# Expert passes of a mixture-of-experts kernel: the first product of small tiles turned round, and the weights of both layers split as two streams

## The chip, the cores and the metric

The kernel runs on one core of a Trainium2 chip. The metric is the device time of the kernel in microseconds; what is compared is the median of several runs.

## What is computed

Three stages, one after another. Attention over windows of 32 queries gives x of 3072 tokens by 512 features. A mixture of experts follows: tokens with x @ w_skip > 0 go through one of 8 experts, the others are left as they are. The last stage takes the largest of three products and multiplies again. The change is in the second stage:

```python
def _moe_ref(x, w_skip, w_gate, w1, w2):
    do_compute = x @ w_skip > 0
    xc = x[do_compute]
    e_idx = np.argmax(xc @ w_gate, axis=1)          # w_gate: 512 x 8
    ...
    for e in range(E):                               # E = 8
        mask = e_idx == e
        h = np.maximum(xc[mask] @ w1[e], 0.0)        # w1[e]: 512 x 1024
        y[mask] = gate_w[mask, None] * (h @ w2[e])   # w2[e]: 1024 x 512
    out[do_compute] = xc + y
```

## The kernel before

Tokens are sorted by expert into tiles of at most 256 tokens (`TOK`). A tile of at most 128 tokens (`P`) is *small*; small tiles come first. With these inputs there are eight tiles: two small ones (passes 0 and 1) and six of 256 (passes 2 to 7). A pass is `tile_pass(i, tokens)`, which every engine has for itself, in a loop over small tiles, in a loop over the large ones, and once more written out for the last tile, where the transposes and sums of the final stage are interleaved.

The precision of fp32 is kept with three products of a rounded part and a rest: `three` issues lo\*hi, hi\*lo and hi\*hi. So every operand is split: ScalarE (ACT) copies it to the reduced type fp32r (`w_hi<-raw`, line 837; `h_hi<-ps_h`, line 851; `x_hi<-ps_x`, line 841), and VectorE (DVE) subtracts that from the original (`w_lo<-raw,w_hi`, line 1215; `h_lo`, line 1267; `x_lo`, line 1222).

A pass has eight feature blocks of 128 hidden features. The weights of block c are one chunk of 128 x 1024 numbers, 512 KB: 512 columns of w1 and 512 of w2. SyncE (SP) loads chunks into a ring of four buffers `raw`; a load waits until DVE has split the chunk four before it. ACT writes the high part when the chunk has landed and TensorE (PE) has used the block four before (`s_used`). The first product of block f (`first_product`) holds w1 in PE and streams the tokens of x past: 4 x 3 matmuls with 128 or 256 columns, result `ps_h`, features by tokens. The second (`second_product`) holds a block of h and streams 512 columns of w2 past: three matmuls for each 128 tokens, result `ps_y`. PE runs one block ahead: first product of f+1, then second product of f. Near the end of a pass PE transposes the x rows of the next tile (`turn`, eight transposes, result `ps_x`).

At the end of a pass DVE adds the result to the old rows (`sums_out`, `x_out<-ps_y,g_nat,x_nat`, line 1279). GpSimd (POOL) waits for that sum (`s_xo`), copies the rows of the next tile (`x_nat<-x_in`, line 656, 128 x 1024 within SBUF), and then issues the gathers of the tile after it and the scatter of the sums.

Of the kernel before, what the change touches and what calls it, by code (L numbers as in the profile page):

```python
# [14 lines left out]
P = 128  # L15
# [38 lines left out]
CHK = KD * P + DM  # L54
RAW = 4
RING = 4
LEAD = 3
# [46 lines left out]
def build(nc, qT, kT, vW, w9, wpack, wunit, wout, out):  # L104
# [8 lines left out]
    with ctx:  # L113
# [54 lines left out]
        with ExitStack() as moe:  # L168
            sb, ps = tensors(moe)

            w_hi = [sb(f"w_hi{i}", [P, CHK], F32R) for i in range(RING)]
            w_lo = [sb(f"w_lo{i}", [P, CHK], F32R) for i in range(RING)]
            raw = sb("raw", [P, RAW, CHK])
# [7 lines left out]
            sb("last_stage", [P, (7 * 2 * KH * HT + UBUF * 8 * KH * P + 2 * 7 * KH * P)])  # L181
# [102 lines left out]


# [68 lines left out]

        s_load = [sem(f"s_load{i}") for i in range(RAW)]
        s_whi = sem("s_whi")
        s_wlo = sem("s_wlo")
# [54 lines left out]
        def w1_part(w, k):  # L412
            return w[:, k * P:(k + 1) * P]

        def w2_part(w):
            return w[:, KD * P:]
# [22 lines left out]
        def _(sp):  # L439
# [42 lines left out]
            def load_chunk(e, c, split=None):  # L482
                if split is not None:
                    sp.wait_ge(s_wlo, split)
                sp.dma_start(raw[:, c % RAW, :], wpack[bass.ds(e, 1), c].rearrange("a p c -> (a p) c"))\
                    .then_inc(s_load[c % RAW], 16)

            for c in range(LEAD):
                load_chunk(e0, c)
# [3 lines left out]
            sp.dma_start(gate_dram.rearrange("(p t) o -> p (t o)", p=P), gate[:, :]).then_inc(s_gst, 16)  # L493
            def load_pass(i):
                e_now = sp.value_load(table[0:1, bass.ds(i, 1)], min_val=0, max_val=E - 1)
                e_next = sp.value_load(table[0:1, bass.ds(i + 1, 1)], min_val=0, max_val=E - 1)
                for c in range(LEAD, FB):
                    load_chunk(e_now, c, i * FB + c + 1)
                for c in range(LEAD):
                    load_chunk(e_next, c, i * FB + FB + c + 1)  # L500
# [9 lines left out]
            for c in range(LEAD, FB):  # L510
                load_chunk(e_last, c, last * FB + c + 1)

            for n in range(2, UBUF):
                load_unit(n)
# [275 lines left out]
        def _(act):  # L790
# [42 lines left out]
            def split_w(i, c):  # L833

                act.wait_ge(s_load[c % RAW], i * (16 * FB // RAW) + 16 * (c // RAW + 1))
                act.wait_ge(s_used, i * FB + c + 1)
                act.activation(w_hi[c % RING][:, :], raw[:, c % RAW, :], ACT.Copy).then_inc(s_whi, 1)  # L837

# [5 lines left out]
            for c in range(LEAD):  # L844
                split_w(0, c)
            act.wait_ge(s_tr, 1)
            split_x(P)

            def hidden_high(i, f, tokens):
                act.wait_ge(s_h, i * FB + f + 1)  # L850
                act.activation(h_hi[f % 2][:, 0:tokens], ps_h[f % 2][:, 0:tokens], ACT.Relu).then_inc(s_hhi, 1)

            def tile_pass(i, tokens):
                for f in range(FB):
                    hidden_high(i, f, tokens)
                    if f == FB - 1:
                        act.wait_ge(s_tr, i + 2)
                        split_x()
                    if f + LEAD < FB:
                        split_w(i, f + LEAD)  # L860
                    else:
                        split_w(i + 1, f + LEAD - FB)

            with act.Fori(0, small) as i:
                tile_pass(i, P)
            unit_high(0)
            with act.Fori(small, rest + SPARE - 1) as i:
                tile_pass(i, TOK)
# [124 lines left out]
            for f in range(FB):  # L993
                hidden_high(last, f, TOK)
                if f + LEAD < FB:
                    split_w(last, f + LEAD)
# [39 lines left out]
        def _(dve):  # L1036
# [155 lines left out]
            dve.sem_inc(s_wlo, RAW)  # L1192
# [20 lines left out]
            def split_w(i, c):  # L1213
                dve.wait_ge(s_whi, i * FB + c + 1)
                dve.tensor_tensor(w_lo[c % RING][:, :], raw[:, c % RAW, :], w_hi[c % RING][:, :].bitcast(F32),  # L1215
                                  ALU.subtract).then_inc(s_wlo, 1)
# [28 lines left out]
            split_w(0, 0)  # L1245
            split_w(0, 1)
            unit_sums(0)
            split_x(0, P)

# [15 lines left out]
            def hidden_low(i, f, tokens):  # L1265
                dve.wait_ge(s_hhi, i * FB + f + 1)
                dve.scalar_tensor_tensor(out=h_lo[f % 2][:, 0:tokens], in0=ps_h[f % 2][:, 0:tokens], scalar=0.0,
                                         in1=h_hi[f % 2][:, 0:tokens].bitcast(F32), op0=ALU.max, op1=ALU.subtract)\
                    .then_inc(s_hlo, 1)

            def sums_out(i, tokens):
                dve.wait_ge(s_nat, i * 2 + 2)
                dve.wait_ge(s_landed, i + 1)
                for t in range(tokens // P):
                    if t == 0 and tokens > P:
                        dve.wait_ge(s_y, i + 1)
                    else:
                        dve.wait_ge(s_used, i * FB + FB + RING)
# [4 lines left out]
            def tile_pass(i, tokens):  # L1283
                for f in range(FB):
                    hidden_low(i, f, tokens)
                    if f == FB - 1:
                        split_x(i + 1)
                    elif f + LEAD < FB:
                        if f == 0:
                            split_w(i, LEAD - 1)  # L1290
                        split_w(i, f + LEAD)
                    else:
                        split_w(i + 1, f + LEAD - FB)
                sums_out(i, tokens)

            with dve.Fori(0, small) as i:
                tile_pass(i, P)
            with dve.Fori(small, rest + SPARE - 1) as i:
                tile_pass(i, TOK)
# [135 lines left out]
            for f in range(FB):  # L1435
                hidden_low(last, f, TOK)
                if f == 0:
                    split_w(last, LEAD - 1)
                if f + LEAD < FB:
                    split_w(last, f + LEAD)  # L1440
# [36 lines left out]
        def _(pe):  # L1477
# [146 lines left out]
            def first_product(i, f, tokens):  # L1624
                pe.wait_ge(s_wlo, i * FB + f + 1 + RAW)
                pe.wait_ge(s_hlo, i * FB + f + 1)
                for k in range(KD):
                    if f == 0 and k % (KD // 2) == 0:
                        pe.wait_ge(s_xlo, i * 2 + k // (KD // 2) + 1)
                    last = three(ps_h[f % 2][:, 0:tokens], w1_part(w_hi[f % RING], k), w1_part(w_lo[f % RING], k),  # L1630
                                 x_hi[:, k, 0:tokens], x_lo[:, k, 0:tokens], k == 0, k == KD - 1)
                last.then_inc(s_h, 1)

            def second_product(i, f, tokens):
                pe.wait_ge(s_hlo, i * FB + f + 3)
# [12 lines left out]
            def tile_pass(i, tokens):  # L1648
                first_product(i, 0, tokens)
# [187 lines left out]
```

## Time and profile before

| what | us |
|---|---|
| median of 3 runs | 673.04 (672.7 to 674.03) |
| the profiled execution | 675.65 |
| its span, first to last instruction | 673.9 |
| attention and routing, up to the first expert matmul | 121.57 |
| expert passes 0 to 7 | 121.57 to 304.50 |
| final stage | 304.50 to 673.90 |

The profiled execution took 675.65 us, 1.75 us more than its span. The granted TensorE clock is 1.000 over the whole span. Line numbers are those of the kernel before. A matmul in the trace has a modelled duration that is longer than the distance to the next one; how fast PE goes is read from the distance between starts.

### The profile page before, as it was taken

What the parts mean: (1) busy time and instruction counts of PE and PEld (TensorE: products, weight loads), DVE (VectorE), ACT (ScalarE), POOL (GpSimd) and SP (SyncE); (2) the same over time, 40 slices, a digit from 0 to 9 for tenths busy, and PEclk for the clock granted to TensorE, in tenths of its full rate; (3) what the DMA queues carried; (4) which work ended last, traced back from release to release, by engine and by line L of the source; (5) the groups of instructions that cost most, each with busy time, mean ns of one, the idle gap of its engine ahead of it and who ended that gap; (6) DMA issues with size and microseconds to landing.
All of it is one profiled execution on the core that took longest, in us unless ns stands there. A gap on an engine that the chain in (4) does not pass through costs nothing.

```text
span 673.9 us, 13069 instructions
## 1 busy us (share of the span) xinstructions
PE 651.8 (97%) x4864; PEld 542.4 (80%) x4864; DVE 460.1 (68%) x820; ACT 318.9 (47%) x504; POOL 174.6 (26%) x210
## 2 busy tenths in 40 slices
PE   4999989999999999999999999999999999999998
PEld 3778865788997999988888888888888888888886
DVE  4778867877666656798899873378889516888500
ACT  4445442556544555564455453345456424445311
POOL 7411222476675375405300012100000220000000
DMA  8999964767675587713601115121101111110011
GB/s 301 410 328 341 344 232 175 262 233 265 199 245 166 180 298 248 234 41 119 214 32 63 62 48 188 47 64 62 63 32 63 59 67 52 44 63 32 0 63 62
DMA packets 32505, 101.07 MB, mean 150 GB/s; under 512 B 6012, under 2 KB 6156, under 8 KB 32336
## 3 DMA queue, kind: packets, MB, share of 16 engines
q1 hardware_dynamic: 26288, 87.12, 37.6%
q0 software_dynamic: 6176, 13.41, 5.7%
q8 instruction: 25, 0.41, 0.2%
q14 instruction: 16, 0.13, 0.1%
HBM read 87.11 MB, written 16.80 MB: 154 GB/s over the span
## 4 chain that ended last, share of the span: by engine, by line
PE 89%; DVE 4%; DMA 2%; issue 2%; ACT 1%; another core or an unknown queue 1%; SPq 1%; DVEq 0%; ACTq 0%
PE ps_c L1620 9%; PE ps_c L1622 9%; PE ps_c L1621 8%; PE ps_b L1622 5%; PE ps_b L1620 5%; PE ps_b L1621 5%; PE ps_s L1490 4%; PE ps_h L1620 4%; PE ps_h L1622 4%; PE ps_h L1621 4%; PE ps_o L1505 4%; PE ps_y L1620 3%; PE ps_y L1621 3%; PE ps_y L1622 3%; PE ps_f L1622 2%; PE ps_f L1620 2%
## 5 line engine op out<-in xcount | busy, mean ns | idle before, releaser
L1215 DVE TENSOR_TENSOR w_lo<-raw,w_hi 128x1024 fp32r<-128x1024 f32 x64 | 79.5, 1254 | 42.1 <-ACT w_hi L837 33.7
L837 ACT ACTIVATE w_hi<-raw 128x1024 fp32r<-128x1024 f32 x64 | 67.8, 1060 | 47.6 <-PE ps_y L1622 26.2
L1238 DVE TENSOR_TENSOR u_lo<-u_f,u_hi 128x1792 fp32r<-128x1792 f32 x27 | 54.6, 2023 | 50.3 <-ACT u_hi L826 50.3
L1620 PE MATMUL ps_c<-c_hi,u_lo 128*128 128x512 f32 x216 | 85.2, 394 | 0.6
L1622 PE MATMUL ps_c<-c_hi,u_hi 128*128 128x512 f32 x216 | 84.2, 390 | 0.0
L1621 PE MATMUL ps_c<-c_lo,u_hi 128*128 128x512 f32 x216 | 84.2, 390 | 0.0
L1620 PE MATMUL ps_h<-x_hi,w_lo 128*128 128x256 f32 (+1 forms) x256 | 71.5, 279 | 1.7 <-DVE w_lo L1215 0.9
L1622 PE MATMUL ps_h<-x_hi,w_hi 128*128 128x256 f32 (+1 forms) x256 | 71.9, 281 | 0.0
L1621 PE MATMUL ps_h<-x_lo,w_hi 128*128 128x256 f32 (+1 forms) x256 | 71.9, 281 | 0.0
L777 POOL DMA_INDIRECT out<-f_out,order x16 | 17.6, 1100 | 207.5 <-ACT f_out L792 206.9
L792 ACT ACTIVATE f_u<-ps_c 128x512 f32<-128x512 f32 x58 | 34.6, 597 | 69.8 <-PE ps_c L1622 67.5
L826 ACT ACTIVATE u_hi<-u_f 128x1792 fp32r<-128x1792 f32 x27 | 46.0, 1702 | 27.8 <-PE ps_c L1622 26.0
L1620 PEld LDWEIGHTS ps_h<-x_hi,w_lo 128*128 128x128 f32 x256 | 48.9, 191 | 6.3 <-DVE x_lo L1222 2.5
L1620 PEld LDWEIGHTS ps_c<-c_hi,u_lo 128*128 128x128 f32 x216 | 40.5, 188 | 13.2 <-ACT f_p L792 4.2
L1621 PEld LDWEIGHTS ps_h<-x_lo,w_hi 128*128 128x128 f32 x256 | 48.9, 191 | 2.0
L1622 PEld LDWEIGHTS ps_h<-x_hi,w_hi 128*128 128x128 f32 x256 | 48.9, 191 | 0.0
L1620 PE MATMUL ps_y<-w_hi,h_lo 128*128 128x512 f32 x112 | 46.1, 412 | 1.7 <-issue 1.3
L1622 PEld LDWEIGHTS ps_c<-c_hi,u_hi 128*128 128x128 f32 x216 | 40.6, 188 | 8.6
L1621 PEld LDWEIGHTS ps_c<-c_lo,u_hi 128*128 128x128 f32 x216 | 40.6, 188 | 8.1
L1621 PE MATMUL ps_y<-w_lo,h_hi 128*128 128x512 f32 x112 | 44.1, 394 | 0.0
L1622 PE MATMUL ps_y<-w_hi,h_hi 128*128 128x512 f32 x112 | 43.8, 391 | 0.0
L1621 PE MATMUL ps_b<-c_lo,u_hi 128*128 128x512 f32 x108 | 42.0, 389 | 0.0
(240 smaller groups left out, 1504.3 us busy)
## 6 DMA issues: line engine op xcount, KB each, us to landing
raw<-wpack SPq DMA_DIRECT2D x64, 512.0 KB
u_f<-wunit SPq DMA_DIRECT2D x27, 512.0 KB, 3.3
v_sb<-vW SPq DMA_DIRECT2D x32, 390.0 KB, 5.3
k_sb<-kT SPq DMA_DIRECT2D x32, 250.0 KB, 4.9
q_sb<-qT SPq DMA_DIRECT2D x16, 384.0 KB, 6.0
x_dram<-x_buf SPq DMA_DIRECT2D x4, 1536.0 KB, 10.2
f_in<-x_dram SPq DMA_DIRECT2D x1, 2048.0 KB, 9.0
out<-f_out SPq DMA_DIRECT2D x8, 256.0 KB, 2.0
```

The costliest lines, as they stand in the source:

```text
L777: pool.indirect_dma_start(out=out[0:LISTED, :], out_offset=bass.IndirectOffsetOnAxis(ap=order[:, n:n + 1], axis=0), in_=f_out[:, t % OUTS, ...
L792: return act.activation(dst, src, ACT.Copy)
L826: act.activation(u_hi[n % 2][:, :, :], u_f[n % UBUF][:, 1:8, :], ACT.Copy).then_inc(s_uhi, 1)
L837: act.activation(w_hi[c % RING][:, :], raw[:, c % RAW, :], ACT.Copy).then_inc(s_whi, 1)
L1215: dve.tensor_tensor(w_lo[c % RING][:, :], raw[:, c % RAW, :], w_hi[c % RING][:, :].bitcast(F32), ALU.subtract).then_inc(s_wlo, 1)
L1238: dve.tensor_tensor(u_lo[n % UBUF][:, 1:8, :], u_f[n % UBUF][:, 1:8, :], u_hi[n % 2][:, :, :].bitcast(F32), ALU.subtract).then_inc(s_ulo, 1)
L1490: last = pe.matmul(ps_s[g % 2][CHUNK * r:CHUNK * (r + 1), t, :, :], q_sb[j][:, c * CHUNK:(c + 1) * CHUNK], k_sb[j][:, :, c * BLOCK:c * BLO ...
L1505: last = pe.matmul(ps_o[g % 2][CHUNK * r:CHUNK * (r + 1), t, :, :], probT[:, t, CHUNK * r:CHUNK * (r + 1)], v_sb[j][:, :, c, :], start=Tru ...
L1620: pe.matmul(out_, a_lo, b_hi, start=first, stop=False, skip_group_check=goes_on)
L1621: pe.matmul(out_, a_hi, b_lo, start=False, stop=False, skip_group_check=goes_on)
L1622: return pe.matmul(out_, a_hi, b_hi, start=False, stop=end, skip_group_check=goes_on)
```

## The change

For small tiles the first product is turned round: x (128 tokens) is held in PE and 256 columns of w1, two feature blocks, stream past (`first_pair`). The result is tokens by features, so ACT writes its relu to `h_nat`, PE transposes it in two steps (`turn_pair`) into a PSUM bank (`h_bank`), and from there it is split into `h_hi` and `h_lo`, for two blocks at once. `second_pair` is the second product of both blocks.

For all tiles the weights come as two streams instead of one: a load brings w1 of a pair of blocks, or w2 of a pair (still 128 x 1024 numbers, 512 KB, eight loads in a pass), each with two raw buffers. The split w1 has room for all four pairs of a pass, the split w2 for two. The order of loads, of splits and of hidden parts is written out by hand for ACT, DVE and SP. Buffers move within SBUF to make room. In the last pass the third load of the final stage's weights waits for a late first product.

The small pass on PE:

```diff
+            def first_pair(i, p):
+                pe.wait_ge(s_w1lo, i * FP + p + 1 + RAW)
+                for k in range(KD):
...
+                    last = three(ps_h[p % 2][:, :].rearrange("p (f c) -> p f c", f=2), x_hi[:, k, 0:P], x_lo[:, k, 0:P],
+                                 w1_hi[p][:, :, at], w1_lo[p][:, :, at], k == 0, k == KD - 1)
+                last.then_inc(s_h, 2)
+            def turn_pair(i, p):
+                pe.wait_ge(s_relu, i * FP + p + 1)
+                for j in range(2):
+                    last = pe.transpose(h_bank(p)[:, j * P:(j + 1) * P], h_nat[p % 2][:, j * P:(j + 1) * P], ident[:, :])
+                last.then_inc(s_ht, 1)
...
+            def small_pass(i):
+                first_pair(i, 0)
+                first_pair(i, 1)
+                turn_pair(i, 0)
+                first_pair(i, 2)
+                turn_pair(i, 1)
+                pe.wait_ge(s_xo, i * TB + TB)
+                second_pair(i, 0)
+                first_pair(i, 3)
+                turn_pair(i, 2)
+                second_pair(i, 1)
+                turn_pair(i, 3)
+                second_pair(i, 2)
+                turn(i + 1)
+                second_pair(i, 3)
```

The small pass and the large pass on DVE, and a load on SP:

```diff
+            def small_pass(i):
+                split_second(i, 1)
+                turned_low(i, 0)
+                split_first(i, 3)
+                turned_low(i, 1)
+                split_first(i + 1, 0)
+                split_second(i, 2)
+                turned_low(i, 2)
+                split_first(i + 1, 1)
+                split_second(i, 3)
+                turned_low(i, 3)
+                split_x(i + 1)
+                sums_out(i, P)
+                split_first(i + 1, 2)
+                split_second(i + 1, 0)
+            def tile_pass(i):
+                hidden_low(i, 0)
+                split_second(i, 1)
+                hidden_low(i, 1)
...
+                hidden_low(i, 7)
+                split_x(i + 1)
+                sums_out(i, TOK)
+                split_second(i + 1, 0)
...
+            def load_second(e, i, p):
+                if not (isinstance(i, int) and p < RAW):
+                    sp.wait_ge(s_w2lo, i * FP + p + 1)
+                sp.dma_start(raw2[:, p % RAW, :, :], wpack[bass.ds(e, 1), 1, p].rearrange("a p c -> (a p) c"))\
+                    .then_inc(s_load2[p % RAW], 16)
```

What stands at the end of a large pass on DVE before, with x_lo the split of the next tile's x and x_out the two sums of the pass:

```order
L1267 SCALAR_TENSOR_TENSOR h_lo<-ps_h,h_hi 128x256
L1221 ISA
L1222 TENSOR_TENSOR x_lo<-ps_x,x_hi 128x512
L1221 REGISTER_ALU
L1222 TENSOR_TENSOR x_lo<-ps_x,x_hi 128x512
L1272 ISA
L1279 SCALAR_TENSOR_TENSOR x_out<-ps_y,g_nat,x_nat 128x512
L1278 REGISTER_ALU
L1279 SCALAR_TENSOR_TENSOR x_out<-ps_y,g_nat,x_nat 128x512
L1298 ISA
L1298 COMPARE_AND_BRANCH
```

And after the change, at the same place:

```order
L1367 SCALAR_TENSOR_TENSOR h_lo<-ps_h,h_hi 128x256
L1319 ISA
L1320 TENSOR_TENSOR x_lo<-ps_x,x_hi 128x512
L1319 REGISTER_ALU
L1320 TENSOR_TENSOR x_lo<-ps_x,x_hi 128x512
L1377 ISA
L1384 SCALAR_TENSOR_TENSOR x_out<-ps_y,g_nat,x_nat 128x512
L1383 REGISTER_ALU
L1384 SCALAR_TENSOR_TENSOR x_out<-ps_y,g_nat,x_nat 128x512
L1313 TENSOR_TENSOR w_lo<-raw,w_hi 128x1024
L1426 ISA
L1426 COMPARE_AND_BRANCH
```

A split of weights (w2 of the next tile's first pair) now stands between the last sum of a pass and the branch back to the first h_lo of the next; before, the first h_lo followed the sum and the splits came behind it.

The start of a small pass on ACT before:

```order
L851 ACTIVATE h_hi<-ps_h 128x128
L835 ISA
L836 REGISTER_ALU
L837 ACTIVATE w_hi<-raw 128x1024
L850 REGISTER_ALU
L851 ACTIVATE h_hi<-ps_h 128x128
L835 REGISTER_ALU
L836 REGISTER_ALU
L837 ACTIVATE w_hi<-raw 128x1024
```

And after, where h_nat is the relu of a pair and h_hi its high part read back from the bank it was turned into:

```order
L883 ACTIVATE w_hi<-raw 128x1024
L903 ISA
L904 ACTIVATE h_nat<-ps_h 128x256
L903 REGISTER_ALU
L904 ACTIVATE h_nat<-ps_h 128x256
L907 REGISTER_ALU
L908 ACTIVATE h_hi<-ps_y 128x256
L877 REGISTER_ALU
L878 ACTIVATE w_hi<-raw 128x1024
```

The first relu of a pass moved behind a split of weights that waits for its load, and each pair now takes ACT two steps with PE's transposes between them.

## Rows read from the trace of the kernel before

**Rows 1.** The page, part 1: busy us (share of the span), instructions

```profile
PE 651.8 (97%) x4864; PEld 542.4 (80%) x4864; DVE 460.1 (68%) x820; ACT 318.9 (47%) x504; POOL 174.6 (26%) x210
```

**Rows 2.** Windows, one per pass: length, then busy us of each engine

```profile
121.57:139.18 17.61, 17.48 (x129) 15.91 (x129) 13.80 (x26) 10.91 (x18) 10.20 (x11) 1.00 0.77 253
139.18:158.30 19.12, 17.91 (x129) 15.92 (x129) 14.29 (x20) 11.20 (x19) 14.39 (x16) 1.00 0.79 268
158.30:181.99 23.69, 23.69 (x153) 21.54 (x153) 15.25 (x21) 14.56 (x20) 17.04 (x17) 1.00 0.70 223
181.99:207.44 25.45, 23.86 (x153) 21.11 (x151) 14.31 (x20) 11.76 (x18) 16.71 (x18) 1.00 0.68 212
...
230.97:254.38 23.41, 23.41 (x153) 21.38 (x152) 15.15 (x21) 12.54 (x18) 15.14 (x15) 1.00 0.74 243
...
277.79:304.50 26.71, 26.59 (x178) 23.96 (x177) 24.85 (x39) 16.34 (x29) 6.35 (x5) 1.00 0.26 88
```

**Rows 3.** Timeline of PE in pass 0: start us, us, instruction

```profile
121.95 0.27 PE L1620 MATMUL ps_h<-x_hi,w_lo 128*128 128x128 f32 x1
...
124.19 0.28 PE L1622 MATMUL ps_h<-x_hi,w_hi 128*128 128x128 f32 x1
...
124.81 0.40 PE L1622 MATMUL ps_y<-w_hi,h_hi 128*128 128x512 f32 x1
125.04 0.23 PE L1620 MATMUL ps_h<-x_hi,w_lo 128*128 128x128 f32 x1
```

**Rows 4.** Timeline of PE in pass 5, and the chain at a turn

```profile
230.97 0.28 PE L1620 MATMUL ps_h<-x_hi,w_lo 128*128 128x256 f32 x1
...
231.92 0.28 PE L1622 MATMUL ps_h<-x_hi,w_hi 128*128 128x256 f32 x1
...
274.34 0.87 PE ps_x L1614 x8
```

**Rows 5.** Groups by form, all passes: xcount, busy us, mean ns, idle before

```profile
L1215 DVE TENSOR_TENSOR w_lo<-raw,w_hi 128x1024 fp32r<-128x1024 f32 x62 | 77.2, 1255 | 40.8 <-ACT w_hi L837 33.7 <-issue 6.8
L1267 DVE SCALAR_TENSOR_TENSOR h_lo<-ps_h,h_hi 128x256 fp32r<-128x256 f32 x48 | 20.0, 417 | 7.8 <-ACT h_hi L851 5.7 <-issue 2.1
L1222 DVE TENSOR_TENSOR x_lo<-ps_x,x_hi 128x512 fp32r<-128x512 f32 x14 | 9.0, 686 | 2.9 <-ACT x_hi L841 2.9
L1279 DVE SCALAR_TENSOR_TENSOR x_out<-ps_y,g_nat,x_nat 128x512 f32<-128x512 f32 x12 | 8.5, 745 | 1.0 <-PE ps_y L1622 1.0
L837 ACT ACTIVATE w_hi<-raw 128x1024 fp32r<-128x1024 f32 x61 | 64.7, 1060 | 42.5 <-PE ps_y L1622 26.2 <-issue 13.3 <-DMA raw<-wpack 3.0
L851 ACT ACTIVATE h_hi<-ps_h 128x256 fp32r<-128x256 f32 x48 | 18.5, 386 | 25.6 <-PE ps_h L1622 21.0 <-remote 3.0 <-issue 1.1
```

**Rows 6.** The page, part 6 (us to landing), and the chain in pass 1

```profile
u_f<-wunit SPq DMA_DIRECT2D x27, 512.0 KB, 3.3
145.00 6.07 DMA raw<-wpack
```

**Rows 7.** Tile w_lo at 141 us; copy of POOL; DVE at 122 us

```profile
L1215 DVE TENSOR_TENSOR w_lo<-raw,w_hi x1: 2415/2415/2415, 141.3 to 141.3; 128x1024 fp32r<-128x1024 f32 x1
141.55 1.06 POOL L656 COPY x_nat<-x_in 128x1024 f32<-128x1024 f32 x1
L656 POOL COPY x_nat<-x_in x8: 1036/1038/1057, 121.6 to 279.0; 128x1024 f32<-128x1024 f32 x8
122.22 0.43 DVE L1256 TENSOR_TENSOR moved<-ahead,oh 128x16 f32<-128x16 f32 x1
```

**Rows 8.** Timeline of DVE and POOL where pass 3 begins

```profile
181.61 1.41 DVE L1279 SCALAR_TENSOR_TENSOR x_out<-ps_y,g_nat,x_nat 128x512 f32<-128x512 f32 x2 [0.27 <-PE ps_y L1622]
184.04 0.42 DVE L1267 SCALAR_TENSOR_TENSOR h_lo<-ps_h,h_hi 128x256 fp32r<-128x256 f32 x1 [1.01 <-ACT h_hi L851]
183.19 1.04 POOL L656 COPY x_nat<-x_in 128x1024 f32<-128x1024 f32 x1 [1.30 <-DVE x_out L1279]
```

**Rows 9.** The chain in pass 3: start us, us, what

```profile
201.61 2.95 another core or an unknown queue
```

More of the change, by code:

```diff
@@ L480, in _, with load_first @@
             e0 = sp.value_load(table[0:1, 0:1], min_val=0, max_val=E - 1)
[L482 to L489, printed above, removed]
+            def load_first(e, i, p):
+                if not (isinstance(i, int) and p < RAW):
+                    sp.wait_ge(s_w1lo, i * FP + p + 1)
+                sp.dma_start(raw1[:, p % RAW, :, :], wpack[bass.ds(e, 1), 0, p].rearrange("a p c -> (a p) c"))\
+                    .then_inc(s_load1[p % RAW], 16)
+            def load_second(e, i, p):
+                if not (isinstance(i, int) and p < RAW):
+                    sp.wait_ge(s_w2lo, i * FP + p + 1)
+                sp.dma_start(raw2[:, p % RAW, :, :], wpack[bass.ds(e, 1), 1, p].rearrange("a p c -> (a p) c"))\
+                    .then_inc(s_load2[p % RAW], 16)
+            load_first(e0, 0, 0)
+            load_first(e0, 0, 1)
+            load_second(e0, 0, 0)
             sp.wait_ge(s_xst, 16 * B)
@@ L509, in _ @@
             e_last = sp.value_load(table[0:1, bass.ds(last, 1)], min_val=0, max_val=E - 1)
[L510 to L514, printed above, removed]
+            load_second(e_last, last, 1)
+            load_first(e_last, last, 3)
+            load_second(e_last, last, 2)
+            load_second(e_last, last, 3)
+            sp.wait_ge(s_h, last * FB + FB - 2)
+            load_unit(2)
             sp.wait_ge(s_landed, rest + SPARE + 1)
@@ L853, in tile_pass @@
[L853 to L862, printed above, removed]
+                act.activation(h_hi[f % 2][:, :], ps_h[f % 2][:, :], ACT.Relu).then_inc(s_hhi, 1)
@@ new lines, in turn_pair, with second_pair @@
+            def turn_pair(i, p):
[3 more added lines that the diff above has]
+                last.then_inc(s_ht, 1)
+            def second_pair(i, p):
+                pe.wait_ge(s_hlo, i * FB + 2 * p + 4)
+                pe.wait_ge(s_w2lo, i * FP + p + 1 + RAW)
+                for j in range(2):
+                    f = 2 * p + j
+                    last = three(ps_y[0][:, :], h_hi[p % 2][:, j * P:(j + 1) * P], h_lo[p % 2][:, j * P:(j + 1) * P],
+                                 w2_part(w2_hi, f), w2_part(w2_lo, f), f == 0, f == FB - 1)
+                last.then_inc(s_used, 1)
+                if p == FP - 1:
+                    pe.sem_inc(s_y, 1)
```

265 lines of the change are left out of this document (180 added, 85 removed).

## Prediction

> **What bounds the kernel now.** I read the page's busy shares first: PE is busy 97% of the span [rows 1], so a change helps if it takes work from PE, and hurts if it makes PE wait. Then the windows, cut at the first matmul of each pass [rows 2]. PE fills a large pass: in pass 5 all 23.41 us, DVE only 15.15 and ACT 12.54. In small pass 0 PE is busy 17.48 of 17.61 us, in pass 1 17.91 of 19.12. DVE is busy 13.8 and 14.3 us there, so only some 4 us stand between PE's bound and the next one. Last I looked at what other engines do where one pass goes over into the next, since there the order of DVE changes.
>
> **What a matmul costs** is read from distances between starts. In a small pass 20 matmuls of 128 columns lie between 121.95 and 124.19: 0.112 us each; a matmul of 512 columns takes 0.23 us [rows 3]. Of 256 columns eight lie between 230.97 and 231.92: 0.119 us [rows 4]. Twice the columns cost almost nothing more. Eight transposes take 0.87 us, 0.109 each [rows 4].
>
> **PE's work in a small pass.** Before: 96 x 0.112 = 10.75 us for the first product, 24 x 0.23 = 5.5 for the second, 0.87 for the turn of the next x, 17.1 in all. After: 48 x 0.12 = 5.76, 5.5, 0.87, and eight transposes of h, 0.87: 13.0. So 4.1 us of PE's work go in each of two passes, 8.2 us in all. That is the most the new product can give if nothing else takes PE's place.
>
> **What takes its place: the splits.** A small pass still splits eight pieces of 128x1024. On DVE these are 8 x 1.25 = 10.0; the four low parts of h now have 256 columns, 4 x 0.42 = 1.7; x_lo 2 x 0.69, one x_out 0.75 [rows 5]: 13.8 us. ACT has 8 x 1.06 for weights and 8 x 0.39 for relu and high part of four pairs [rows 5], 11.6, with x_hi on top. So DVE alone is above PE's 13.0.
>
> Beyond the busy time stands the way of a buffer. Four raw buffers serve eight loads, so each goes round twice in a pass: load, ACT's split, DVE's split, next load. A load of 512 KB lands in 3.3 us where little else moves, and took 6.07 us in pass 1 [rows 6]. The trace shows no mean for this load; I take the middle of the two, 4.7, since the gathers of POOL lie in each pass. ACT and DVE work in order, so a split waits for what stands ahead of it: half of one other split and one h step, (1.06 + 0.39)/2 = 0.7 on ACT and (1.25 + 0.42)/2 = 0.85 on DVE. One round is 4.7 + 1.06 + 1.25 + 1.55 = 8.56 us, two are 17.1: nearly what pass 0 takes now. The first relu of the pass also stands behind two splits that wait for their loads, and SP loads the second w2 pair only after its two reads of the expert table; I count this as inside the round.
>
> **The copy of POOL.** One more thing lengthens DVE. `w_lo` subtracts two tensors in SBUF. Once, at 141.3, it took 2.415 us instead of 1.25, and in this time, from 141.55, ran POOL's copy of x rows, 1.06 us long [rows 7]. The small subtraction at 122.22 (both inputs in SBUF, 16 columns) took 0.43 us and ended at 122.65, when the copy that began at 121.6 ended [rows 7]. So a subtraction from SBUF stands still while POOL copies; it costs 1.16 us. The Trainium skill says so too (SBUF — State Buffer, section Who interferes with whom): a DVE instruction with two SBUF inputs contends with a GpSimd instruction that reads SBUF, and the loser is blocked for the whole instruction.
>
> POOL copies once in a pass, when the last x_out is done. Before, DVE was then idle: in pass 3 x_out ends at 183.02, the copy runs from 183.19 to 184.23, and DVE does nothing for 1.01 us and then h_lo from 184.04, which reads PSUM [rows 8]. That idle time hid the copy. After the change a w_lo stands right behind x_out, and would begin 0.2 us ahead of the copy, just as the stretched one did. Its high part is there by then, since ACT has nothing between x_hi and it.
>
> Small passes: pass 0 17.1; pass 1, with a copy under a split, 17.1 + 1.16 = 18.3. Together 35.4 against 36.73 [rows 2]: **-1.3**. Ends: with landings of 3.3 us a round is 7.2, the passes 14.3 and 15.5, -6.9; with 6.07 a round is 9.9, the passes 19.9 and 21.0, +4.2.
>
> **Large passes 3 to 7.** Count from the moment E in which PE ends a pass (181.99 for pass 3, [rows 2]). The sums end at E + 1.03 [rows 8]. Then comes the stretched split, 2.41, and h_lo, 0.42 [rows 5]; neighbours on DVE overlap by 0.08 (two x_out of 0.745 take 1.41 [rows 5, 8]), so h_lo is ready at E + 3.70. PE does two first products meanwhile, 24 x 0.12 = 2.88 us, and then needs h_lo for the second product. Before it came at E + 2.47 (184.04 + 0.42). PE now waits 3.70 - 2.88 = 0.82 us, in five passes: **+4.1**. Nothing gives this back, as PE fills the rest of the pass. Without the stretch h_lo is ready at E + 2.54 and the term is 0.
>
> **Pass 2** follows a small pass, where DVE has two splits behind the sum: 1.03 + 2.41 + 1.25 + 0.42 - 0.24 = E + 4.87, a wait of **+2.0** (0.8 without the stretch).
>
> **The last pass** takes 26.71 us where PE is busy with 22.6 (8 x 2.82; 2.82 is 12 x 0.12 + 6 x 0.23) and 32 transposes, 3.5: 0.6 us are lost to DVE and ACT. Two of their splits move to the pass ahead, so I give **-0.5** (0 to -0.6). The load of the final stage that is put later has until the third unit of that stage, 3.3 us against more than 20. The other loads of large passes are asked for more than half a pass ahead: 0. The moved SBUF buffers: 0.
>
> **Sum:** -1.3 + 2.0 + 4.1 - 0.5 = +4.3 us. Against the profiled execution's own 675.65 that is 679.95. That execution has a gap in pass 3, which took 25.45 where pass 5 took 23.41 [rows 2], with ACT waiting 2.95 us for something the profile does not know [rows 9]; the median of the runs, 673.04, is 2.6 lower. The change has nothing to do with that gap, so I forecast the median: 673.04 + 4.3 = **677.3 us**, slower.
>
> **Rivals.**
>
> A: the forecast, 675 to 680. Chance 0.50.
>
> B: the copy waits for the split, not the split for the copy. Then 2 x 17.1 = 34.2, -2.5; pass 2 +0.8; passes 3 to 7 nothing; last pass -0.5: -2.2, 670.8 us, **faster**. It decides at each pass's start: h_lo before or after E + 2.88. For it: `w_lo` would start first. Against it: the one at 141.3 started first too and was stretched, while the copy kept its 1.04 in all eight passes [rows 7]. Chance 0.15. The Trainium skill speaks for this rival (same page and section): whichever of the two starts first has the ports for its whole instruction. By that rule the time would be that of B; the stretched row speaks against it.
>
> C: loads land early, as with 3.3 us, the copy stretches as forecast: -6.9 + 2.0 + 4.1 - 0.5 = -1.3, 671.7 us; half of this case's values, with landings between, end above 673. For it: in large parts of the passes DMA is at 0.77 share [rows 2], not full. Chance 0.15. With B as well: 666 to 669, chance 0.06.
>
> D: loads land late, shorter passes ask for the same 4 MB and the gathers in less time: +4.2 + 2.0 + 4.1 = +10.3, up to 683. Chance 0.14.
>
> **Numbers.** What a measurement tells from no change is 0.2%, 1.35 us. Slower: A 0.50, D 0.13: 0.63. Faster: B 0.13, C 0.07, both 0.06: 0.26. Within: 0.11. The range takes in A, B, most of C and the lower part of D: 670.5 to 681.
>
> **What the profile after would show.** First products of small passes at 0.12 us a matmul and 48 of them; transposes of h_nat at 0.109. Small passes of some 17 and 18 us, PE waiting in them for h_lo, ACT for loads. A `w_lo` of 2.2 to 2.4 us at the start of each large pass, over POOL's copy, and PE waiting 0.8 us for h_lo there. Passes 3 to 6 of 24.2 us instead of 23.4. I am wrong if that `w_lo` takes 1.25 us, or if small passes come under 16 us.

## The result and the profile after

The change takes 676.5 us (median of 20 executions; the kernel before 674.08 beside it). The ratio is 1.0047, with an interval of 1.0035 to 1.0059: slower by 2.4 to 4.0 us, 3.2 in the middle. The forecast was +4.3. The ratios here leave out the executions of some 684 us and more, of which the kernel before had 5 of 20 (673.7 is the median of its other 15), the change none, and `old_small` below 8 of 12 (687 to 694); what they are is not known.

The page of the change, part 1, answers to [rows 1]:

```profile
PE 645.4 (96%) x4784; PEld 536.8 (80%) x4784; DVE 464.4 (69%) x812; ACT 316.4 (47%) x504; POOL 173.6 (26%) x210
```

PE has 80 matmuls and 6.4 us of busy time less, and the kernel is slower. Where this went is told by the windows, cut as in [rows 2] at each pass's first matmul (length, busy us of each engine, granted clock, DMA share, GB/s); the last row is the final stage:

```profile
121.61:138.68 17.07, 13.88 (x88) 12.04 (x89) 13.65 (x22) 12.23 (x19) 10.23 (x13) 1.00 0.75 254
138.68:157.21 18.53, 15.74 (x89) 13.86 (x88) 13.84 (x15) 12.28 (x20) 11.47 (x12) 0.87 0.81 300
157.21:182.42 25.21, 24.56 (x154) 22.31 (x152) 17.14 (x21) 12.68 (x19) 16.86 (x17) 0.96 0.69 229
182.42:205.83 23.41, 23.41 (x153) 21.39 (x152) 15.54 (x21) 11.74 (x18) 15.27 (x14) 1.00 0.62 216
...
276.26:303.44 27.18, 26.32 (x178) 23.91 (x176) 24.08 (x38) 16.62 (x29) 5.29 (x5) 1.00 0.24 85
303.44:674.10 370.66, 365.76 (x1631) 299.74 (x1629) 243.89 (x372) 163.43 (x241) 31.60 (x26) 1.00 0.19 68
```

Against [rows 2]: passes 0 and 1 together 35.60 for 36.73 (-1.13), pass 2 25.21 for 23.69 (+1.52), passes 3 to 6 not longer (23.41, 23.61, 23.41, 23.41; before they took 25.45 with its gap, 23.53, 23.41, 23.41), the last pass 27.18 for 26.71 (+0.47), the final stage 370.66 for 369.40 (+1.26). Together, and without the gap of 2.04 us in pass 3 of the execution before, that is +2.2 us. The forecast's largest term, +4.1 in passes 3 to 7, is not there. Two others that it had at -0.5 and 0 are +0.5 and +1.3.

PE's waits, from its timeline (start, length, instruction, idle time ahead of it and what ended it):

```profile
137.19 0.50 PE L1752 MATMUL ps_y<-w_hi,h_lo 128*128 128x512 f32 x1 [1.88 <-DVE h_lo L1373]
155.07 0.50 PE L1752 MATMUL ps_y<-w_hi,h_lo 128*128 128x512 f32 x1 [2.77 <-DVE h_lo L1373]
161.78 0.50 PE L1752 MATMUL ps_y<-w_hi,h_lo 128*128 128x512 f32 x1 [0.65 <-DVE h_lo L1367]
301.93 0.50 PE L1752 MATMUL ps_y<-w_hi,h_lo 128*128 128x512 f32 x1 [0.86 <-DVE h_lo L1367]
326.85 0.50 PE L1752 MATMUL ps_c<-c_hi,u_lo 128*128 128x512 f32 x1 [1.13 <-ACT f_p L834]
```

The first two are the ends of the small passes, the third is in pass 2, the fourth in the last pass, the fifth in the final stage. Shorter waits in the small passes are left out. No such wait stands in passes 3 to 6.

**Who waits at a pass's start.** DVE and POOL where pass 3 begins, which answers to [rows 8], and where pass 2 begins:

```profile
182.05 1.41 DVE L1384 SCALAR_TENSOR_TENSOR x_out<-ps_y,g_nat,x_nat 128x512 f32<-128x512 f32 x2 [0.26 <-PE ps_y L1754]
183.37 1.22 DVE L1313 TENSOR_TENSOR w_lo<-raw,w_hi 128x1024 fp32r<-128x1024 f32 x1
184.50 0.42 DVE L1367 SCALAR_TENSOR_TENSOR h_lo<-ps_h,h_hi 128x256 fp32r<-128x256 f32 x1
183.62 1.87 POOL L698 COPY x_nat<-x_in 128x1024 f32<-128x1024 f32 x1 [3.69 <-DVE x_out L1384]
...
158.20 1.22 DVE L1308 TENSOR_TENSOR w_lo<-raw,w_hi 128x1024 fp32r<-128x1024 f32 x1
159.33 2.06 DVE L1313 TENSOR_TENSOR w_lo<-raw,w_hi 128x1024 fp32r<-128x1024 f32 x1
158.44 1.87 POOL L698 COPY x_nat<-x_in 128x1024 f32<-128x1024 f32 x1 [2.55 <-DVE x_out L1384]
```

In pass 3 the split keeps its 1.22 us and the copy is the one that is stretched, from 1.04 to 1.87: rival B's mechanism (pass 5 is alike, 1.22 and 1.86). h_lo is ready at 184.92 = E + 2.50, ahead of the need at E + 2.88. In pass 2 two splits follow each other. The first keeps 1.22 and the copy waits for it; then the copy runs to 160.31 and the second split, begun at 159.33, waits for the copy and ends at 161.39. Each waits for the one that began before it. The Trainium skill says this (SBUF — State Buffer, Who interferes with whom): whichever of the two is issued first has the ports for its whole instruction; these rows agree.

In passes 4, 6 and 7 these two did not meet at all: the copy began 3.3, 4.1 and 2.4 us into the pass, when the split behind the sum had ended. In pass 4 it met a later split, and the picture of [rows 7] came back. First that split of the kernel before, then pass 4 of the change, then pass 4 of loads_swapped, a kernel of the experiments below:

```profile
141.28 2.42 DVE L1215 TENSOR_TENSOR w_lo<-raw,w_hi 128x1024 fp32r<-128x1024 f32 x1
141.30 0.22 POOL L694 COPY idx_s<-idx 128x2 int32<-128x2 int32 x1
...
208.83 2.40 DVE L1313 TENSOR_TENSOR w_lo<-raw,w_hi 128x1024 fp32r<-128x1024 f32 x1 [0.49 <-ACT w_hi L883]
208.85 0.21 POOL L736 COPY idx_s<-idx 128x2 int32<-128x2 int32 x1
209.09 1.04 POOL L698 COPY x_nat<-x_in 128x1024 f32<-128x1024 f32 x1
...
207.48 1.22 DVE L1313 TENSOR_TENSOR w_lo<-raw,w_hi 128x1024 fp32r<-128x1024 f32 x1
207.51 1.22 POOL L736 COPY idx_s<-idx 128x2 int32<-128x2 int32 x1
```

Two small copies of POOL stand directly ahead of the large one (the second, of 0.21 and 0.19 us, is not shown). In the first two places the split's record begins 0.02 us ahead of the first small copy, and yet the split waits. It ends 1.09 us behind the large copy (143.70 for 142.61, 211.23 for 210.13), as the second split of pass 2 does, which surely came after the copy (161.39 for 160.31, 1.08 us). So its subtraction ran when the three copies were over: there POOL had come first and kept its place over all three. In loads_swapped the split's record leads by 0.03 us, and there the split keeps 1.22 us and the small copy is stretched from 0.21 to 1.22. A split that begins between two small copies can also get in between them: in pass 3 of old_small it began at 186.30, 0.10 us behind the first and 0.03 us ahead of the second, and kept 1.21 us, while the second copy took 1.22. So starts that lie this close do not show who came first, and the stretched split of [rows 7] is no clear case against the rule. What decides there was read from the traces, not tried by an edit, and stays open.

The lost split costs little where it stands: pass 4 takes 23.60 to 23.62 us in the six kernels in which the split took 2.40 us there (the change, small_end, last_final, short_loads, short_splits, best2), and 23.41 in loads_swapped and best3, where it did not.

**The granted clock** fell, which the forecast had not seen. Windows of 2 us of the change:

```profile
136.00:138.00 2.00, 0.81 (x4) 0.68 (x5) 1.86 (x4) 2.00 (x4) 1.68 (x4) 1.00 0.25 87
138.00:140.00 2.00, 2.00 (x11) 1.87 (x10) 1.60 (x3) 0.78 (x1) 0.12 (x1) 0.68 0.96 334
140.00:142.00 2.00, 2.00 (x11) 2.00 (x11) 2.00 (x2) 1.44 (x2) 1.74 (x1) 0.50 0.45 178
154.00:156.00 2.00, 0.93 (x4) 0.74 (x5) 1.86 (x4) 2.00 (x4) 1.34 (x3) 0.94 0.53 201
156.00:158.00 2.00, 2.00 (x8) 1.71 (x7) 0.91 (x2) 2.00 (x2) 0.00 (x0) 0.50 0.84 297
```

After each of the two long waits the clock goes from 2.4 to 1.2 GHz (0.50) for a few us. What this cost had to be tried.

### The profile page after: what moved, and what is told of

It reads as the page before. It is cut to its first block, busy times and chain, and to the rows that moved or that the text cites. A ratio compares the mean times of both kernels' runs of the same rounds, so it can differ in the third digit from the quotient of the medians.

```text
span 674.1 us, 12987 instructions
## 1 busy us (share of the span) xinstructions
PE 645.4 (96%) x4784; PEld 536.8 (80%) x4784; DVE 464.4 (69%) x812; ACT 316.4 (47%) x504; POOL 173.6 (26%) x210
## 4 chain that ended last, share of the span: by engine, by line
PE 86%; DVE 4%; DMA 4%; issue 3%; ACT 1%; SPq 1%; POOL 0%; DVEq 0%; ACTq 0%; POOLq 0%
PE ps_c L1752 8%; PE ps_c L1753 8%; PE ps_c L1754 8%; PE ps_b L1752 5%; PE ps_b L1754 5%; PE ps_b L1753 5%; PE ps_s L1622 4%; PE ps_y L1752 4%; PE ps_o L1637 4%; PE ps_h L1754 3%; PE ps_h L1753 3%; PE ps_h L1752 3%; PE ps_y L1753 3%; PE ps_y L1754 3%; PE ps_f L1752 2%
## 5 line engine op out<-in xcount | busy, mean ns | idle before, releaser
L1754 PE MATMUL ps_h<-x_hi,w_hi 128*128 128x256 f32 x192 | 54.7, 285 | 0.0
L1753 PE MATMUL ps_h<-x_lo,w_hi 128*128 128x256 f32 x192 | 54.7, 285 | 0.0
L1752 PE MATMUL ps_h<-x_hi,w_lo 128*128 128x256 f32 x192 | 54.6, 284 | 0.0
L1313 DVE TENSOR_TENSOR w_lo<-raw,w_hi 128x1024 fp32r<-128x1024 f32 x32 | 42.2, 1322 | 10.9 <-ACT w_hi L883 10.6
L1308 DVE TENSOR_TENSOR w_lo<-raw,w_hi 128x1024 fp32r<-128x1024 f32 x32 | 39.6, 1241 | 13.4 <-ACT w_hi L878 11.8
L899 ACT ACTIVATE h_hi<-ps_h 128x256 fp32r<-128x256 f32 x48 | 18.4, 384 | 64.2 <-PE ps_h L1754 63.6
L1752 PE MATMUL ps_b<-c_hi,u_lo 128*128 128x512 f32 x108 | 42.0, 389 | 0.0
L1754 PE MATMUL ps_b<-c_hi,u_hi 128*128 128x512 f32 x108 | 42.0, 389 | 0.0
```

What stands on the lines that cost most here:

```text
L899: act.activation(h_hi[f % 2][:, :], ps_h[f % 2][:, :], ACT.Relu).then_inc(s_hhi, 1)
L1308: dve.tensor_tensor(w1_lo[p][:, :, :], raw1[:, p % RAW, :, :], w1_hi[p][:, :, :].bitcast(F32), ALU.subtract).then_inc(s_w1lo, 1)
L1313: dve.tensor_tensor(w2_lo[p % RING][:, :, :], raw2[:, p % RAW, :, :], w2_hi[p % RING][:, :, :].bitcast(F32), ALU.subtract).then_inc(s_w2lo, 1)
L1752: pe.matmul(out_, a_lo, b_hi, start=first, stop=False, skip_group_check=goes_on)
L1753: pe.matmul(out_, a_hi, b_lo, start=False, stop=False, skip_group_check=goes_on)
L1754: return pe.matmul(out_, a_hi, b_hi, start=False, stop=end, skip_group_check=goes_on)
```

## Experiments

All were timed against the kernel before on the same chip; "ratio" is of that. Pass lengths are from one profile each, in us. Alike code gives small passes that differ by over 1 us from profile to profile (35.60, 35.56 and 34.28 in the change, split_after_copy and last_final).

| kernel | ratio (interval) | passes 0+1 | pass 2 | passes 3 to 6 | last | final stage |
|---|---|---|---|---|---|---|
| before | 1 | 36.73 | 23.69 | 23.41 to 25.45 | 26.71 | 369.40 |
| the change | 1.0047 (1.0035 to 1.0059) | 35.60 | 25.21 | 23.41 to 23.61 | 27.18 | 370.66 |
| loads_swapped | 1.0065 (1.0042 to 1.0088) | 35.91 | 25.57 | 23.41 to 23.42 | 27.15 | 370.85 |
| warm | 1.0039 (1.0022 to 1.0056) | 37.59 | 25.21 | 23.42 to 24.86 | 27.17 | 370.30 |
| old_small | 1.0035 (1.0000 to 1.0071) | 37.89 | 23.67 | 23.41 to 24.94 | 27.16 | 370.55 |
| split_after_copy | 1.0108 (1.0085 to 1.0131) | 35.56 | 25.19 | 24.54 to 25.61 | 27.17 | 371.36 |
| large_order | 1.0117 (1.0087 to 1.0148) | 35.56 | 25.24 | 24.36 to 24.37 | 27.15 | 370.44 |
| small_end | 1.0034 (1.0014 to 1.0055) | 34.02 | 24.74 | 23.41 to 23.60 | 27.78 | 370.59 |
| last_final | 1.0019 (1.0000 to 1.0038) | 34.28 | 25.18 | 23.41 to 23.61 | 26.21 | 369.28 |
| best1 | 1.0076 (1.0047 to 1.0105) | 34.92 | 25.54 | 24.35 to 24.37 | 26.21 | 369.23 |
| short_loads | 0.9976 (0.9962 to 0.9991) | 31.91 | 25.17 | 23.41 to 23.62 | 27.17 | 371.27 |
| short_splits | 0.9990 (0.9968 to 1.0013) | 34.99 | 24.34 | 23.41 to 23.61 | 27.29 | 370.20 |
| best2 | 0.9999 (0.9982 to 1.0016) | 36.09 | 24.42 | 23.41 to 23.60 | 26.84 | 369.29 |
| best3 | 1.0001 (0.9985 to 1.0018) | 34.42 | 24.25 | 23.41 to 23.42 | 26.20 | 369.27 |

**loads_swapped**, on SP:

```diff
-                load_first(e_next, i + 1, 1)
                 load_second(e_now, i, 3)
+                load_first(e_next, i + 1, 1)
```

> The change, but SP asks for w2 of pair 3 ahead of w1 of the next tile's pair 1. In the profile after the change that w2 load of pass 1 left SP at 146.80, though its buffer was free when the split of pair 1's w2 ended, some 2.8 us earlier; it landed at 152.26 and PE waited 2.77 us for the h_lo behind it (1.88 us in pass 0). Theory 1 (the order of the loads makes the waits, and the falls of the granted clock follow the waits): both waits shrink to under 0.7 us, the clock stays at 1.00 between 138 and 160, passes 0 and 1 take 15 to 16.5 us each and pass 2 24.1, the time falls by 4 to 6 us to some 671 to 672. Theory 2 (bandwidth and DVE bind, the order only moves the wait to the next load): the sum of passes 0 to 2 changes by under 1 us, 676.

The wait at the end of pass 1 fell from 2.77 to 0.59 us, but waits of 0.93 and 0.88 us for h_nat and h_lo came ahead of it, the one of pass 0 stayed (1.73), and the sum is not shorter. Theory 1 falls: the order of the loads is not what binds.

**warm**, on PE in a small pass:

```diff
                 turn(i + 1)
+                for _ in range(16):
+                    pe.transpose(h_bank(2)[:, 0:P], ident[:, :], ident[:, :])
                 second_pair(i, 3)
```

> The change, with 16 transposes of the identity into an unused bank ahead of the second product of pair 3 in small passes (16 x 0.109 = 1.75 us of PE work, inside waits of 1.88 and 2.77 us). The waits themselves stay. Theory 1 (the granted clock fell to half because PE stood idle there, and the fall costs 2 to 3 us at the starts of passes 1 and 2): no level of half after either wait, passes 1 and 2 together shorter by 2 to 3 us, some 674. Theory 2 (the falls have another cause, or cost nothing as PE has slack in small passes): 676.5 within 0.7 us.

The long wait at the end of pass 1 is gone (waits of 1.13 and 0.88 us stand ahead of it), and the clock did not fall there; after pass 0, where 2.10 us of waiting remained, it did. Two windows of warm, the fall and pass 2, and pass 2 of last_final, in whose expert passes the clock never fell:

```profile
140.00:142.00 2.00, 2.00 (x8) 1.65 (x7) 1.12 (x3) 0.93 (x1) 1.47 (x2) 0.60 0.79 262
159.99:185.20 25.21, 23.72 (x153) 21.45 (x152) 16.53 (x20) 12.97 (x19) 17.70 (x17) 1.00 0.71 240
```

```profile
157.79:182.97 25.18, 23.68 (x154) 21.44 (x152) 17.14 (x21) 13.35 (x20) 16.79 (x17) 1.00 0.72 244
```

Pass 2 takes 25.2 us whether the clock is 0.96 (the change) or 1.00. At full clock PE is done earlier and then waits 1.5 us for h_lo instead of 0.65. DVE sets that moment, so the fall cost nothing there. Pass 1, too, takes 18.33 us in last_final without a fall and 18.53 in the change with one. Theory 1 falls; the time is that of the change within its uncertainty.

**old_small** gives the functions of the large pass a width, on PE, ACT and DVE, and runs small tiles through them, as on PE:

```diff
-                    last = three(ps_h[f % 2][:, :], w1_part(w1_hi, f, k), w1_part(w1_lo, f, k),
-                                 x_hi[:, k, :], x_lo[:, k, :], k == 0, k == KD - 1)
+                    last = three(ps_h[f % 2][:, 0:tokens], w1_part(w1_hi, f, k), w1_part(w1_lo, f, k),
+                                 x_hi[:, k, 0:tokens], x_lo[:, k, 0:tokens], k == 0, k == KD - 1)
...
             with pe.Fori(0, small) as i:
-                small_pass(i)
+                tile_pass(i, P)
```

> The two streams and all orders of the large pass, with small tiles computed the way of before (w1 held, 128 columns of x past, no turn of h). Theory 1 (the turned product is worth its 1 to 2 us in the small passes but loses about as much to waits and clock): small passes of 17.3 and 18.5 us bound by PE, no fall of the clock, pass 2 24.1; the time is that of the change within 1 us, 676 to 677. Theory 2 (the two streams themselves cost nothing and the turned product is what loses): 674. Theory 3 (the streams are what loses): 677.5 or more, as the saved PE work is gone too.

Closest to theory 1, though the interval is wide. The small pass of the change saves 2.3 us (35.60 for 37.89) and loses 1.5 in pass 2 (25.21 for 23.67); it ends with two splits behind the sum on DVE and the one of old_small with one. That is 0.8 us by these profiles, too little for the ratios to tell. The two streams alone bring the longer last pass and the longer final stage.

**split_after_copy**, on DVE at the end of a large pass:

```diff
                 sums_out(i, TOK)
+                dve.wait_ge(s_nat, i * 2 + 3)
                 split_second(i + 1, 0)
```

> The change, but at the end of a large pass DVE waits for POOL's copy of x rows before it splits w2. This makes by hand what the prediction took for granted, a split that is late by the copy. The prediction's arithmetic: h_lo at E + 3.70 or later against a need at E + 2.88, so passes 3 to 7 longer by 0.8 us or more each, 4 us or more in all, 680.5 or above. The other reading (the slack at a pass's start is larger than 0.82 us short, so the copy never mattered): 676.5 within 0.7 us.

Pass 5 of this kernel, with DVE and POOL at its start:

```profile
234.68:259.22 24.54, 23.67 (x153) 21.43 (x152) 15.61 (x21) 11.74 (x18) 14.94 (x15) 1.00 0.68 234
```

```profile
236.97 1.23 DVE L1313 TENSOR_TENSOR w_lo<-raw,w_hi 128x1024 fp32r<-128x1024 f32 x1 [1.25 <-POOL x_nat L698]
235.90 1.04 POOL L698 COPY x_nat<-x_in 128x1024 f32<-128x1024 f32 x1 [11.08 <-DVE x_out L1384]
```

24.54 for 23.41, +1.13: a split that waits for the copy costs what the prediction said and a little more. PE waits 0.87 us there, where the forecast had 0.82. In passes 3 and 4 it is more (25.05 and 25.61). The last pass stays at 27.17, as 16 transposes for the final stage stand there ahead of the first second product. So the arithmetic of the slack was right for passes 3 to 6; what was wrong is who waits.

**large_order**, on DVE:

```diff
             def tile_pass(i):
                 hidden_low(i, 0)
+                split_second(i, 0)
                 split_second(i, 1)
...
                 sums_out(i, TOK)
-                split_second(i + 1, 0)
```

(and the same move in the small pass and the last one.)

> The change, but on DVE the split of the next tile's first w2 pair goes back behind the first h_lo of the next pass, as before the change. Theory 1 (POOL's copy waits for the split, a large pass starts without a wait; only pass 2, where two splits stand ahead of the first h_lo, pays): passes 3 to 6 stay at 23.41 us, pass 2 falls from 25.2 by 1.1 us, in all about 1 us faster than the change, ratio to before 1.003. Theory 2 (the prediction's term: the split behind the sum costs 0.8 us at each large pass): passes 3 to 7 shorter by 0.8 each than those of the change.

Both expectations are wrong. A window of its pass 4, one of PE's waits, POOL's copy:

```profile
208.61:232.98 24.37, 23.65 (x154) 21.44 (x153) 15.53 (x21) 11.74 (x18) 11.07 (x13) 1.00 0.58 199
```

```profile
187.99 0.47 PE L1752 MATMUL ps_y<-w_hi,h_lo 128*128 128x512 f32 x1 [0.72 <-DVE w_lo L1313]
185.44 1.04 POOL L698 COPY x_nat<-x_in 128x1024 f32<-128x1024 f32 x1 [3.68 <-DVE x_out L1383]
```

The copy is back at 1.04 us, as nothing stands against it. But the first second product needs the w2 split of its own pair, which now comes behind h_lo: PE waits for it, and each large pass is 0.96 us longer. With w1 and w2 in separate streams this split has to stand ahead of h_lo.

**best1** put the order of large_order together with the edits of small_end and last_final, which follow. It was expected at 0.998 to 1.001 and came out at 1.0076, a miss, as the loss of large_order comes with it. Its large passes take 24.35 to 24.37 us, each with a wait of 0.72 us for w_lo, as in large_order.

**small_end**, on DVE:

```diff
                 split_x(i + 1)
-                sums_out(i, P)
                 split_first(i + 1, 2)
+                sums_out(i, P)
                 split_second(i + 1, 0)
```

> The change, but at the end of a small pass DVE splits w1 of pair 2 ahead of the sum, in the 1.1 us in which it waits for PE, and only the w2 split stays behind the sum. Theory 1 (pass 2 is 1.5 us longer than before because of DVE's queue ahead of the first h_lo): pass 2 falls by 1.1 to 1.5 us to some 23.9, pass 1 by 0 to 0.5; ratio to before 1.002 to 1.003. Theory 2 (pass 2 is long for the fall of the granted clock): pass 2 stays at 25.2 where the clock falls.

Pass 2 falls by 0.5 us, to 24.74, less than the 1.1 to 1.5 expected, while the clock is 0.94 in it. With the same order it is 24.42 in best2 (clock 0.95) and 24.25 in best3 (1.00). So DVE's queue is a cause. Once it is shorter, the clock seems to cost something, 0.2 to 0.5 us by these single profiles; best3 has its loads in another order too. Even there 0.6 us of the loss against 23.69 are left. The last pass has one more wait of PE here, 0.40 us for a load of x rows, as in best2 and not in best3.

**last_final**, on SP, and on ACT and DVE alike:

```diff
             load_unit(2)
+            sp.wait_ge(s_prod, 7)
+            load_unit(UBUF)
             sp.wait_ge(s_landed, rest + SPARE + 1)
             sp.dma_start(o_f[:, :, :], wout).then_inc(s_oload, 16)
...
             for f in range(FB):
+                if f == 5:
+                    split_second(last, 3)
                 hidden_high(last, f)
...
-                if f == 5:
-                    split_second(last, 3)
```

> The change, with two edits behind pass 6: in the last pass ACT and DVE split w2 of pair 3 ahead of the sixth relu instead of behind it, and SP asks for the fourth unit of the final stage ahead of the output weights (1.5 MB) instead of behind them. Theory 1 (the last pass is 0.46 us longer since that split moved back, and PE waits 1.13 us in the final stage for a copy that is queued on ACT behind the unit's late landing): last pass 26.6 instead of 27.17, no wait for f_p at 326, final stage 369.4 to 369.6 instead of 370.7; 1.6 us less in all, ratio to before 1.002. Theory 2 (PE's two waits only move): under 0.5 us.

The chain of the change in the last pass and in the final stage (start, us, what) shows what these edits are aimed at:

```profile
292.63 1.06 ACT w_hi L883
...
293.72 1.23 DVE w_lo L1313
...
301.55 0.34 DVE h_lo L1367
...
310.48 3.79 DMA x_dram<-x_out,idx_s
...
314.72 8.21 DMA u_f<-wunit
...
326.22 0.59 ACT f_p L834
```

The windows of last_final:

```profile
276.81:303.02 26.21, 26.21 (x177) 23.90 (x176) 24.24 (x38) 15.67 (x27) 5.28 (x5) 1.00 0.28 92
303.02:672.30 369.28, 365.45 (x1631) 299.64 (x1629) 244.29 (x372) 164.45 (x243) 29.97 (x26) 1.00 0.20 68
```

Both waits are gone: 0.97 us in the last pass and 1.38 in the final stage. The ratios agree (1.0047 to 1.0019 is 1.9 us). The edits ran together; that the first gave the one and the second the other is read from where the time went.

**short_loads** and **short_splits** take work away in the loop over small tiles:

```diff
-                load_first(e_next, i + 1, 0)
+                half_first(e_next, i + 1, 0)
...
-                split_first(i + 1, 0)
+                short_first(i + 1, 0)
```

(the first line pair in short_loads, the second in short_splits; six of eight in each). short_loads leaves out the second half of each of these chunks, short_splits the low part of half the columns of each of these splits on DVE.

> The change, but in the loop over small tiles six of the eight loads of a pass bring 256 KB instead of 512 (the second half of each of these chunks is not loaded). All splits and products stay as they are. Theory 1 (the way of a buffer binds: load, two splits, next load): a landing is 1.5 us or more shorter, pass 0 and pass 1 take 14 to 15 us each, near DVE's 13.8. Theory 2 (ACT's and DVE's order binds): 16.5 us or more.

> The change, but in small passes six of the eight w_lo splits of DVE do only 128 of 1024 columns (most of the low part is left out), which takes some 0.3 instead of 1.22 us: 5.5 us of DVE's 13.8 us of a pass are gone. Theory 1 (DVE's work binds a small pass): passes 0 and 1 shorter by 3 us or more. Theory 2 (the loads bind): a buffer comes free 1 us earlier, but the transfers take as long; under 1.5 us shorter.

Windows of passes 0 and 1, of short_loads and then of short_splits:

```profile
123.42:139.13 15.71, 13.62 (x89) 11.99 (x90) 13.55 (x22) 11.92 (x19) 9.83 (x10) 1.00 0.51 173
139.13:155.33 16.20, 13.79 (x89) 11.98 (x88) 13.61 (x15) 11.71 (x19) 12.76 (x14) 1.00 0.68 228
```

```profile
121.43:139.45 18.02, 14.40 (x89) 12.52 (x90) 10.08 (x22) 12.12 (x19) 9.95 (x11) 0.96 0.77 261
139.45:156.42 16.97, 14.80 (x90) 13.18 (x88) 7.93 (x15) 11.60 (x19) 10.98 (x15) 0.90 0.87 305
```

And the landings of the loads between 121 and 158 us, in the change (first row) and in short_loads (count, KB each, us to landing):

```profile
raw<-wpack SPq DMA_DIRECT2D x16, 512.0 KB, 4.7
```

```profile
raw<-wpack SPq DMA_DIRECT2D x7, 512.0 KB, 4.2
raw<-wpack SPq DMA_DIRECT2D x12, 256.0 KB, 3.4
```

With six of eight loads halved, the landings of the halves are 1.3 us shorter and the two passes 3.7 us (35.60 to 31.91), 4.8 us in all by the ratios, with some 1.3 either way. With a third of DVE's work away (27.5 to 18.0 us) the two passes are 0.6 us shorter in the profile and pass 2 by 0.9, as its short splits stand in DVE's queue too; the ratios say 3.8 us, with some 1.7 either way. So both the loads and DVE's splits lie on the way of a buffer. By the profiles the loads weigh more; the ratios do not tell the two apart. DVE's busy time alone does not bind: in short_loads the passes take 15.71 and 16.20 us with DVE busy 13.6. How the rest divides between the order of ACT and that of DVE is left open.

**best2** and **best3** put the helpful edits together, without the order of large_order.

> The change with the edits that helped: w1 pair 2 split ahead of the sum in small passes; in the last pass w2 pair 3 split ahead of the sixth relu; the fourth unit of the final stage asked for ahead of the output weights. The w2 split stays behind the sum. From the runs of the single edits: small passes 34, pass 2 24.2 to 24.7, passes 3 to 6 23.41, last pass 26.2, final stage 369.3; ratio to before 1.0034 + 1.0019 - 1.0047 = 1.0006. If edits share one gain: 1.002.

> The kernel of best2, with SP asking for w2 of pair 3 ahead of w1 of the next tile's pair 1 as well. With DVE's queue at the end of a small pass shortened, the earlier load may show what it could not before: PE's wait for h_lo at the end of pass 1 (3.4 us) falls to under 1 us. If transfers bind as a whole, the wait moves on to the next load and the ratio stays that of best2 within 0.001; if only the order bound, 2 us less, 0.998.

Both stand at the time of before, within 0.2%. The swapped loads of best3 again give nothing (1.0001 for 0.9999 in best2), and its wait at the end of pass 1 is 2.74 us. best3 in windows, pass 2, the last pass and the final stage:

```profile
157.42:181.67 24.25, 23.68 (x153) 21.43 (x152) 16.79 (x22) 13.58 (x20) 17.17 (x19) 1.00 0.77 252
275.33:301.53 26.20, 26.20 (x178) 23.90 (x177) 23.72 (x38) 15.68 (x27) 6.19 (x5) 1.00 0.24 76
301.53:670.80 369.27, 365.45 (x1631) 299.71 (x1629) 244.18 (x372) 164.56 (x243) 29.97 (x26) 1.00 0.20 68
```

What the change lost is won back, and nothing more. No version that does all of the work beats the kernel before by what a measurement can tell.

## Why the prediction came out as it did

The sign was right, and 677.3 us is close to 676.5. That it is so close is luck: the largest term is not there, and losses that the forecast had at nothing or as a gain made up for half of it. By its own steps:

- **Small passes, -1.3.** Measured -1.13 in the profile. PE's first products did fall to 48 matmuls a pass, and PE's busy time from 17.48 to 13.88 us in pass 0 and from 17.91 to 15.74 in pass 1, part of which ran at half the clock. Of these 5.8 us 1.1 us remain as time. The step said that what takes PE's place is the way of a raw buffer. short_loads shows that the loads are on it and that DVE's 13.8 us alone do not bind. The landing of 4.7 us that it assumed is the median measured; it was the middle of two values, so this agreement is in part luck, and the passes of alike kernels scatter by as much as the term.
- **Pass 2, +2.0.** Measured +1.52, by the mechanism given: two splits behind the sum. The last of them took 2.06 us and not 2.41, as the copy was partly done when it came. Six kernels with this order show 25.2 to 25.6 us; small_end and short_splits, which shorten DVE's queue there, show 24.74 and 24.34. In large_order, with one split ahead of h_lo and one behind, it stays at 25.24, for there PE waits for the split of w2.
- **Passes 3 to 7, +4.1.** This step failed, in the sentence "so a subtraction from SBUF stands still while POOL copies". Where the split behind the sum met the copy, in passes 3 and 5, it came first, kept 1.22 us, and POOL stood still (1.87 and 1.86 us for 1.04); in passes 4, 6 and 7 the copy came when it had ended. The term is 0, but for 0.2 us that a later, stretched split cost in pass 4. That a late split would have cost this much is shown by split_after_copy (+1.13 a pass in passes 5 and 6). Even so the count of five passes was one too many, as the last pass did not grow there. The text had given its own test, "I am wrong if that w_lo takes 1.25 us", and by that test the reason was wrong. It had taken one stretched row over a rule. It saw that the split led the large copy by 0.27 us, and did not ask what else POOL did in that time: two small copies stood in between, the first 0.02 us behind the split.
- **Last pass, -0.5.** Measured +0.47. The step counted splits that leave the pass, not the place of the one that stays. ACT does the last w2 split behind the sixth relu, 16.4 us into the pass (292.63), and from there the chain runs on DVE alone to PE's wait at 301.93. Ahead of that relu it costs nothing: 26.21 us in last_final, which is the -0.5 of the forecast.
- **Final stage, 0.** Measured +1.26, from a wait of 1.13 us. The load put later is not the one: it landed before 296. It is the one after, issued behind 1.5 MB of output weights, with 8.21 us to landing; ACT's f_p stands behind it. The nine kernels here that ask for it behind the output weights wait 0.6 to 1.7 us there; the four that ask earlier (last_final, best1, best2, best3) do not wait. Why the kernel before did not wait stays open. It too asks for this load behind the output weights; there the load had landed 18.1 us after the end of the last pass, here after 19.5, and its only profile can't tell chance from cause.

So +4.3 was made of a term of 4.1 that is not there and of three terms that are 1.0, 1.3 and 0.2 too low, with one 0.5 too high. The profile's own balance is +2.2; the remaining 1 us of the measured 3.2 has no place, and small passes alone scatter by over 1 us from profile to profile.

Of the rivals, B had the mechanism right wherever split and copy met, and its time wrong (670.8): it too had -0.5 and 0 for the last pass and the final stage. C and D did not happen; the landings were in the middle.

## What to carry to other kernels

Work taken from the busiest engine is worth only the distance to the next bound, and here the way of a load buffer stood some 1 us behind PE: ask first what a pass takes if PE's work is nothing. When splits or loads are put in another order, follow the one that stays latest, into the passes and the stage behind; all three losses (pass 2, the last pass, the final stage) were there. And a row that speaks against a rule is worth one more look at what else the other engine did at that moment.

## What was not expected of the hardware

- DVE's subtraction with both inputs in SBUF and POOL's copy take turns whole: copy 1.87 for 1.04 us when the split (1.22) began 0.25 us earlier, split 2.06 us when the copy was under way. Who came first can't be read from starts 0.02 us apart: such splits lost (2.40 us) in the kernel before, in the change and in five more profiles, and one with a lead of 0.03 us won. h_lo, which reads PSUM and one tile of SBUF, kept its 0.42 us beside the copy.
- PE's granted clock was at 1.2 GHz for a few us after single waits of 1.9 to 3.4 us, but not after 2.78 in last_final nor 2.48 and 2.74 in best3, and it fell in stretches with waits of 0.93 and 0.88 (loads_swapped) and of 1.40 and 0.88 (split_after_copy). Where another engine sets the end, this costs nothing (pass 2: 25.21 with it, 25.18 without).
